# Moving the weight product 2.9 places forward in a hand-ordered attention and gating kernel

## The reference

```python
# 1. attention, 8 heads of 64: 32 heads in all
cum  = cumsum(max(s, 0)); bias = -(cum[:, None] - cum[None, :])
attn = softmax(causal(q @ k.T / 8 + min(bias, 0)));  x = attn @ v
# 2. gated block, d_model 512, 5 taps of a causal convolution
gate = sigmoid(sum_k conv_w[k] * x[t - 4 + k])
x    = (gate * (x @ w_val)) @ w_out
# 3. spatial gating, d_ff 1024
h = relu(x @ w_in); u, v = halves(h); v = layernorm(v)
out  = (u * (w_spatial @ v + b_spatial)) @ w_out2
```

## Time and profile before

| what | value |
|---|---|
| median of 3 runs | 500.76 us |
| the runs | 500.76, 502.48, 498.81 us |
| span of the profiled execution | 499.8 us |
| PE busy | 473.0 us, 95% of the span |
| DVE busy | 353.0 us, 71% |
| ACT busy | 333.5 us, 67% |
| POOL busy | 240.2 us, 48% |

### The profile page before, as it was taken

One profiled execution on the slowest core, in us unless ns is written; L12 is line 12 of the kernel. 1 busy time (PEld: TensorE's weight loads), 2 busy tenths in 40 slices (PEclk: granted clock), 3 DMA queues, 4 the chain that ended last, 5 costly groups with the idle time before them and its releaser, 6 DMA issues.

```text
span 499.8 us, 10128 instructions
## 1 busy us (share of the span) xinstructions
PE 473.0 (95%) x3280; PEld 439.9 (88%) x3280; DVE 353.0 (71%) x826; ACT 333.5 (67%) x884; POOL 240.2 (48%) x239
## 2 busy tenths in 40 slices
PE   1699899789999999999999999999999999999997
PEld 1587687579889899999889999999889999998997
DVE  7777879997578968776577867786577877555240
ACT  5798888966887657767777757766777666333322
POOL 4676564453897355335677465225766441112000
PEclk9999999979999999999999999999999999999999
DMA  6775454752543313552353323453333300200002
GB/s 197 218 194 157 119 145 129 209 146 51 139 121 72 97 50 95 145 145 63 89 138 78 92 71 81 114 141 98 97 97 96 72 14 34 74 2 2 0 2 95
DMA packets 46566, 49.73 MB, mean 100 GB/s; under 512 B 24817, under 2 KB 29073, under 8 KB 46514
## 3 DMA queue, kind: packets, MB, share of 16 engines
q1 hardware_dynamic: 46514, 49.09, 37.1%
HBM read 25.82 MB, written 4.95 MB: 62 GB/s over the span
## 4 chain that ended last, share of the span: by engine, by line
PE 74%; DVE 9%; SPq 4%; POOL 4%; issue 4%; ACT 2%; DMA 2%; DVEq 0%; POOLq 0%; ACTq 0%
PE mix L1042 40%; PE attn_o L1010 8%; PE turned L1001 7%; PE score L1042 4%; PE attn_o L1042 4%; PE score L980 3%; PE score L981 3%; DVE u_t L896 2%; DVE prob L859 2%; PE score L988 1%; DMA raw<-in_k 1%; PE score L987 1%; DVE pt_lo L868 1%; PE mix L1116 1%; SPq L535 1%
## 5 line engine op out<-in xcount | busy, mean ns | idle before, releaser
L724 ACT ACTIVATE pt_hi<-turned 128x128 fp32r<-128x128 f32 (+4 forms) x160 | 65.5, 433 | 62.7 <-PE turned L1001 61.9
L859 DVE CUSTOM_DVE_ANT_0 prob<-score,mask_b 128x128 f32<-128x128 f32 (+4 forms) x159 | 80.7, 534 | 22.3 <-PE score L988 17.3
L715 ACT ACTIVATE prob<-prob,neg_max 128x128 f32<-128x128 f32 (+4 forms) x160 | 95.0, 599 | 0.7 <-DVE neg_max L859 0.5
L868 DVE TENSOR_TENSOR pt_lo<-turned,pt_hi 128x128 fp32r<-128x128 f32 (+4 forms) x160 | 73.9, 482 | 29.5 <-ACT pt_hi L724 28.6
L434 POOL TENSOR_TENSOR act_b<-u_t,act_b 128x288 fp32r<-128x288 f32 x48 | 41.3, 863 | 83.5 <-ACT act_b L794 83.4
L1001 PE MATMUL turned<-ident,prob 128*128 128x128 f32 (+1 forms) x480 | 67.7, 271 | 4.6 <-DVE pt_lo L868 3.1
L1010 PE MATMUL attn_o<-pt_hi,v_hl 128*128 128x256 f32 (+2 forms) x224 | 62.4, 298 | 5.5 <-DVE x_t L876 5.4
L1001 PEld LDWEIGHTS turned<-ident,prob 128*128 128x128 f32 (+1 forms) x480 | 55.3, 144 | 12.5 <-ACT prob L715 6.5
L618 POOL TENSOR_TENSOR q<-raw,raw_hi 64x576 fp32r<-64x576 f32 x31 | 45.9, 1480 | 41.2 <-ACT raw_hi L694 39.5
L980 PE MATMUL score<-k,q 68*128 68x256 f32 (+2 forms) x128 | 47.0, 377 | 12.5 <-DMA k<-k 10.2
L896 DVE SCALAR_TENSOR_TENSOR u_t<-x_t,taps,u_t 128x576 f32<-128x576 f32 x64 | 57.8, 903 | 1.4
(11 more groups left out here) (160 smaller groups left out, 975.1 us busy)
## 6 DMA issues: line engine op xcount, KB each, us to landing
q<-raw_hi SPq DMA_DIRECT2D x62, 144.0 KB
k<-raw_hi SPq DMA_DIRECT2D x62, 144.0 KB
r_bc<-r_dram SPq DMA_DIRECT2D x32, 144.0 KB, 3.3
out<-work SPq DMA_DIRECT2D x32, 144.0 KB, 2.2
raw<-in_q SPq DMA_DIRECT2D x31, 144.0 KB, 2.7
raw<-in_k SPq DMA_DIRECT2D x31, 144.0 KB, 2.9
v_raw<-in_v SPq DMA_DIRECT2D x32, 128.0 KB, 2.7
u_t<-in_moe_w_in SPq DMA_DIRECT2D x7, 256.0 KB, 3.3
```

Of the source, the lines that this page charges most:

```text
L715: act.activation(prob_view(i), prob_view(i), ACT.Exp, bias=neg_max[p][0:rows[i], i:i + 1], scale=-1.0, accum_out=row_sum[p][0:rows[i], i:i ...
L724: act.activation(pt_view(pt_hi, i), turned_view((g + i) % 2, i), ACT.Copy).then_inc(pt_hi_done, 1)
L859: dve.tensor_tensor_reduce(prob_view(i), score_view(g, i), mask_b[0:rows[i], at:at + width[i]], -SCALE, -LEAST, ALU.add, ALU.min, neg_max[ ...
L868: dve.tensor_tensor(pt_view(pt_lo, i), turned_view((g + i) % 2, i), pt_view(pt_hi, i).bitcast(F32), ALU.subtract).then_inc(pt_lo_done, 1)
```

## The change

One constant is smaller by 2.9. The 32 parts stood at places 9.4 to 41.73 and stand at 6.5 to 38.83. The evictions move with them: tile 0's from 14.78 to 11.88 on DVE, tile 7's from 43.98 to 41.08, and on ACT from 14.98 to 12.08 and from 44.18 to 41.28. No call is added or removed, and all other calls keep their places.

```diff
-COMB_FROM, COMB_PACE = 9.4, 1.043
+COMB_FROM, COMB_PACE = 6.5, 1.043
```

## The result

The changed kernel takes 501.66 us (median of 20 runs, 500.66 to 502.74), the kernel before 499.70 in the runs beside it (20 runs, 498.13 to 502.48). The ratio is 1.0038, with a 95% interval of 1.0024 to 1.0053: 1.9 us slower, between 1.2 and 2.7. By the bound of 1% that is no change; by the interval it is a small loss. The profiled execution of the changed kernel has a span of 500.1 us and a time of its own of 501.99, so a time lies 1.9 us above its span (1.8 to 2.2 in the 20 runs), not 0.96 as I had it.

What follows compares the result with a forecast made beforehand. PE was taken as full in nearly every slice from 30 us, DVE leading from 73 us until 111.78; +2.1 +0.1 -0.2 -0.4 -0.5 -0.1 -0.7 +0.7 gave +1.0 us, so 501.7 us, range 498.7 to 505.3.

Steps and rivals of the forecast that it cites:

- the most likely class: Whole kernel: a time within 1% of before, given a chance of 0.86.
- The start: PE from about 28 us: three more parts ahead, 2.1 us, plus 0.1 us waiting for piece 7; PE 2.0 us late.
- Which gaps take it up: PE's waits from 39.73 to 61.29 us: they cut its lateness to 1.6, then 1.1 us, passed on to DVE.
- The loan of 2.1 us: PE does three parts' work early, between about 28 and 31 us, and gets the time back where it idles.
- The evictions on DVE: DVE from 74 us: each costs 0.68 us; tile 7's now stands ahead of combine(7), making that about 1.0 us late.
- The sum: All terms for parts, piece 7 wait, gaps and evictions together: +1.0 us, bounds 0 or minus 0.9 below, 2.8 or 4.2 above.
- The wait for `x_hi(3)`: DVE behind combine(7): waits 1.1 to 1.3 us for ACT's x_hi(3), where it waited 0.57 us before.
- The pairing: DVE: tile 4's eviction leaves ahead of the taps at 74 us, minus 0.7; tile 7's comes ahead of combine(7), plus 0.7.
- The clock: PE near 95 us: a gap of about 3 us may lower the clock earlier, but later waits cover it; cost nothing.
- Rival C: PE's clock falls in the new gap and comes back later, 3.5 us on top of 1.0: 505.3 us; chance 0.09.
- The signs: Trace times to settle the cases: combine(7) at 100.3 us confirms, 99.3 or earlier means B, over 101.5 means A.
- rival B: DVE and ACT set the pace and parts go where there is room: 0 to -0.9 us, 500.2 us; chance 0.20.

Runs made afterwards that it cites:

- eviction 7 back: Changed kernel with tile 7's eviction returned to its old place behind combine(7) (43.98 on DVE, 44.18 on ACT); 500.62 us, ratio 1.0007.
- eviction 7 between: Changed kernel with tile 7's eviction at 43.3 on DVE (43.5 on ACT), behind the taps but ahead of combine(7); 501.13 us, ratio 1.0025.
- `x_hi(1)` first: Changed kernel with ACT's x_hi(1) one call ahead of the high parts of weight pieces 16 and 17; 501.28 us, ratio 1.0027.

## Why the prediction was right, and where it was not

The range (498.7 to 505.3), the most likely class and the direction held, and the median, 501.7 against 501.66, agrees by luck, through two errors that cancel. My base was 500.76 us, the median of three runs, where 20 gave 499.70; and my shift was +1.0 us where +1.9 was measured. Step by step:

- **The start** was right. Forecast: first part at about 28 us, part 0.3 at 32, `pv_first(1)` 1.9 us late, wait for piece 7 of 0.1 us within 0 to 1.4. Measured: 27.63, 32.06, 1.78 and 0.31.
- **Which gaps take it up** is the step that failed. I let PE be 1.6 us late at 41 us and 1.1 at 74. It was 0.58 late at `pv_first(2)`, because rows without an idle time held stalls (0.80 us for 0.49), and at 75.25 it was ahead of both traces of before (77.47 and 75.84). The loan of 2.1 us didn't reach the end: with all parts forward and eviction 7 back, the ratio is 1.0007, 0.4 us, between -0.4 and +1.1.
- **The evictions on DVE**: the mechanism was right and the term too small. Eviction 7 ahead of `combine(7)` was put at 0.68 and costs 0.60 itself, plus 0.5 to 0.7 net for POOL, since the tap behind it now meets POOL's operation (1.20) and the pair of taps no longer does (0.65): 1.1 us in the traces, 1.5 by the ratios. The sum had no term for POOL, and says "SP and POOL keep their order". The order was kept; but POOL's operation, 0.35 us behind the start of the tap before, is 0.01 us ahead of it now. The wait for `x_hi(3)` was forecast at 1.1 to 1.3 us and is 1.16.
- **The pairing** of minus 0.7 for tile 4's eviction and plus 0.7 for tile 7's wasn't tested alone. With the loan absorbed, PE and ACT set DVE's pace up to 89.6 us (a wait of 0.94 us on DVE in the changed kernel), so what left the queue ahead of that may have been worth nothing.
- **The clock**: the new gap was forecast at 2.5 to 3.5 us and is 2.92, the clock fell in it, and PE's waits covered it in the profiled execution. That with the clock kept up one falls at 111 us, and that this costs 1.3 us, I hadn't seen. Rival C, a lower clock that lasts ten us longer and costs 3.5, didn't happen: the stretch is 10.2 us long for 6.8, and the way from `combine(7)` to the `val` eviction is 11.97 us for 11.95.
- **The signs** at the end couldn't decide. `combine(7)` was forecast at 100.3 us, with 99.3 or earlier for rival B, and the third `val` product at 112.8; measured were 99.56 and 112.03. But two executions of before have `combine(7)` at 99.33 and 97.66, so a time counted from the start of the span was no sign. Only distances within the stage were.

What stays open: the traces show 1.1 us of the 1.9. The other 0.8 lies within the interval (0.1 to 1.6). The parts themselves (0.4, by the kernel with eviction 7 back) and second falls of the clock in some runs are what could hold it; no run here divides them. The exchange of meetings with POOL is shown in the traces alone: the two kernels that avoid the new meeting (eviction 7 between, `x_hi(1)` first) are not clearly faster than the changed one.

## What to carry to other kernels

Ask of a moved operation first on which side of the hand-off it stands: behind `combine(7)` the eviction lay in a wait and cost nothing, ahead of it it cost all its length, though it was done earlier. Then look who else works when it and its followers run, since here a shift of 0.36 us between DVE and POOL made a tap meet a POOL operation, at 1.2 us, and another shift undid a meeting that had cost 0.65 us unseen. And take a second trace before explaining a difference of 1 us: of two executions of the kernel before, one was 1.7 us later at 90 us.

## What the runs showed of the hardware that was not expected

- DVE and POOL: a tap (128 x 576, one operand) took 1.71 us beside a POOL operation of 1.40 that started 0.01 us ahead of it, and 0.51 without such a meeting; a pair of taps with two operands 2.38 for 1.73; three `x_lo` 3.31 for 2.08. When DVE was first, POOL's operation took 2.43 us for 1.3. DVE operations that read PSUM for one input kept their length (0.62 and 0.74 us).
- PE's granted clock fell to 0.50 at 111 us in the kernel whose clock was kept at 1.00 before, after waits of 1.47 and 2.21 us, and stayed there for about 3.4 us, at 1.3 us of time. In another kernel it fell there after a wait of 1.64, in a third it didn't after 2.19.
- Groups of matmuls without an idle time in their row can hold stalls: three transposes 0.80 us, and 0.49 where PE was late, at a granted clock of 1.00 in both.
